# An attention and feed-forward kernel: the first w3 tile in two halves, and two w3 tiles multiplied with each quarter of wo

## The reference

```
def reference(q, k, v, centroids, moe_x..., moe2_x...):      # q, k, v: (2, 8, 768, 64)
    q_assign = argmax(norm(q) @ norm(centroids).T)           # 16 clusters per head
    k_assign = argmax(norm(k) @ norm(centroids).T)
    scores = where(q_assign == k_assign, q @ k.T / 8, -1e9)
    x = softmax(scores) @ v                                  # -> (1536, 512)
    h = ((x @ w1) * (x @ w2)) @ w3                           # w1, w2: (512, 1024), w3: (1024, 1024)
    x = h @ w_out                                            # w_out: (1024, 512), "wo" in the kernel
    h = x @ w_in                                             # (512, 2048)
    return (max(h, 0) + alpha * min(h, 0)) @ w_out2          # (1536, 512)
```

## Time and profile before

| | us |
|---|---|
| median of 3 runs | 747.94 (747.90 to 747.99) |
| the profiled execution, whole | 747.64 |
| its span, first to last instruction | 745.8 |
| PE busy in the span | 739.0 (99%) |
| DVE, ACT, POOL busy | 411.8, 311.6, 179.5 |

### The profile page before, as it was taken

How to read it: one execution, slowest core, us unless ns; L and a number is a source line. 1 busy time by engine, 2 the same in 40 slices (tenths; PEclk the granted TensorE clock), 3 DMA queues, 4 the chain that set the end, 5 groups by cost and what they waited for, 6 DMA issues and landing times.

```text
span 745.8 us, 10690 instructions
## 1 busy us (share of the span) xinstructions
PE 739.0 (99%) x3792; PEld 641.6 (86%) x3792; DVE 411.8 (55%) x632; ACT 311.6 (42%) x623; POOL 179.5 (24%) x211
## 2 busy tenths in 40 slices
PE   8999999999999999999999999999999999999998
PEld 6888999999999998888888888888888888888886
DVE  4435999999999984721311432575434333343432
ACT  5235988988988884311211422432012111121111
POOL 2141566866865893500000000000000000000000
PEclk9999999999999999999999999999999999999999
DMA  9636366566566233300000022140001000010001
GB/s 293 195 94 144 78 152 155 124 146 154 127 146 153 65 84 92 98 29 1 1 0 1 20 93 85 57 130 11 1 0 57 1 0 1 1 56 1 1 0 57
DMA packets 65371, 54.17 MB, mean 73 GB/s; under 512 B 32032, under 2 KB 54576, under 8 KB 65328
## 3 DMA queue, kind: packets, MB, share of 16 engines
q1 hardware_dynamic: 65328, 53.59, 27.9%
HBM read 31.50 MB, written 3.19 MB: 47 GB/s over the span
## 4 chain that ended last, share of the span: by engine, by line
PE 97%; DVE 1%; DMA 1%; ACT 1%; issue 0%; SPq 0%; DVEq 0%; ACTq 0%
PE slot L625 63%; PE acc L625 24%; PE slot L689 9%; PE acc L638 1%; PE slot L737 1%; DMA early<-in_moe_w_out 1%; DVE xl L1163 0%; DVE xl L1145 0%; ACT xh L938 0%; ACT xh L945 0%; DVE abx L1283 0%; DVE ab L1279 0%; ACT abx L1055 0%; ACT asb L1041 0%; ACT ost L1108 0%
## 5 line engine op out<-in xcount | busy, mean ns | idle before, releaser
L625 PE MATMUL slot<-xh,w 128*128 128x512 f32 x768 | 248.0, 389 | 0.0
L625 PEld LDWEIGHTS slot<-xh,w 128*128 128x128 f32 x768 | 144.1, 188 | 29.8
L625 PE MATMUL slot<-xl,w 128*128 128x512 f32 x384 | 149.4, 389 | 0.0
L1101 ACT CAST gh<-gf 128x512 fp32r<-128x512 f32 x48 | 29.9, 623 | 203.2 <-PE acc L625 186.0
L1206 DVE TENSOR_TENSOR pl<-slot,ph 128x384 fp32r<-128x384 f32 x192 | 97.6, 549 | 8.5 <-ACT ph L973 8.2
L1200 DVE TENSOR_REDUCE nm<-slot 128x1 f32<-128x768 f32 x96 | 91.4, 952 | 15.4 <-PE slot L625 13.8
L973 ACT CAST ph<-slot 128x384 fp32r<-128x384 f32 x192 | 83.5, 489 | 34.3 <-PE slot L689 33.8
L965 ACT ACTIVATE pf<-slot,nm 128x768 f32<-128x768 f32 x96 | 88.4, 921 | 4.6 <-DVE nm L1200 4.5
L625 PEld LDWEIGHTS slot<-xl,w 128*128 128x128 f32 x384 | 72.1, 188 | 15.0
L625 PE MATMUL slot<-k,q 80*128 80x384 f32 (+1 forms) x384 | 82.9, 337 | 0.0
L1329 DVE TENSOR_TENSOR gl<-gf,gh 128x512 fp32r<-128x512 f32 x48 | 33.2, 692 | 89.9 <-ACT gh L1101 89.9
(11 more groups left out here) (121 smaller groups left out, 1012.0 us busy)
## 6 DMA issues: line engine op xcount, KB each, us to landing
stage<-in_moe_w SPq DMA_DIRECT2D x16, 256.0 KB, 3.5
stage<-in_moe_w_in SPq DMA_DIRECT2D x16, 256.0 KB, 2.7
stage<-in_moe_w_out SPq DMA_DIRECT2D x16, 256.0 KB, 3.0
stage<-in_moe_w SPq DMA_DIRECT2D x6, 512.0 KB, 4.2
qk<-in_q SPq DMA_DIRECT2D x16, 192.0 KB, 3.9
qk<-in_k SPq DMA_DIRECT2D x16, 192.0 KB, 3.9
vn<-in_v SPq DMA_DIRECT2D x16, 192.0 KB, 3.8
q<-k SPq DMA_DIRECT2D x16, 192.0 KB, 3.8
```

What stands on the lines that cost most here:

```text
L625: return nc.tensor.matmul(o, a, b, start=start, stop=stop)
L1101: copy(gh[j % 2][:, :], gf[j % 2][:, :]).then_inc(gh_done, 1)
```

## The change

SP loads the first 512 columns of w3 tile 0 first of all, then the centroids, wo quarter 0, the other 512 columns, w3 tile 1, wo quarters 1 to 3, alpha, and the rest as before. PE turns tile 0 in two halves (`turn_first`), ACT and DVE split each half by itself (`first_hi_part`, `first_lo_part`), and ACT rounds wo quarter 0 in two instructions (`wo_first_hi`) with a semaphore of its own on the first. PE multiplies tile 0 with quarter 0, turns the second half and tile 1, and then multiplies tiles 0 and 1 with each quarter in turn. The transposes of the centroids and alpha move in front of the last quarter, and the scaling of the centroids on ACT behind the first rounding work. POOL clears `cwin` before it makes `ident`. There are 6 + 5 spins in place of 8 + 6.

```diff
--- before.py
+++ after.py
@@ -207,6 +207,8 @@
         low_in, join_in = ([sem(f"{name}{e}") for e in range(2)] for name in ("low_in", "join_in"))
         setup_pool, setup_act = sem("setup_pool"), sem("setup_act")
         cen_turned, table_done = sem("cen_turned"), sem("table_done")
+        ld_first, first_turned, first_hi, first_lo = (sem(name) for name in ("ld_first", "first_turned", "first_hi", "first_lo"))
+        wo_first = sem("wo_first")
         piece_hi, piece_lo = sem("piece_hi"), sem("piece_lo")
         front_hi, front_lo = sem("front_hi"), sem("front_lo")
         w3_turned, w3_hi, w3_lo = sem("w3_turned"), sem("w3_hi"), sem("w3_lo")
@@ -239,7 +241,7 @@
         NWO = NF // 2
         READY_W12, READY_W34 = NWO - W12_EARLY, NWO - W12_EARLY + NF
         W3_STAGED = 3
-        IDENT, ZEROS, OPERANDS = 2, 3, 5
+        ZEROS, IDENT, OPERANDS = 1, 3, 5
 
         def staged(e, piece):
 
@@ -381,13 +383,14 @@
                 if c % T6 == 4 and (not last or c // T6 + 2 < HB):
                     next_v(it, c // T6 + 2)
 
+            sp.dma_start(stage[0][:, 0:512], w3d[0][:, 0:512]).then_inc(ld_first, 16)
             sp.dma_start(cn[:, :], cen.rearrange("h c d -> (h c) d")).then_inc(ld_cen, 16)
-            load_w3(0, 0)
             load_wo(0)
-            sp.dma_start(al16, alpha.rearrange("(j p) -> j p", p=P)).then_inc(ld_al, 16)
+            sp.dma_start(stage[0][:, 512:1024], w3d[0][:, 512:1024]).then_inc(ld_stage[0], 16)
+            load_w3(1, 1)
             for i in range(1, NWO):
                 load_wo(i)
-            load_w3(1, 1)
+            sp.dma_start(al16, alpha.rearrange("(j p) -> j p", p=P)).then_inc(ld_al, 16)
             for f in (2, 3):
                 sp.dma_start(early[NWO + f - 2][:, :], w3d[f]).then_inc(ld_early[NWO + f - 2], 16)
             load_qk(0, 0)
@@ -453,10 +456,10 @@
                 ins.then_inc(setup_pool, 1)
                 pool.wait_ge(setup_pool, count[0])
 
+            ordered(nc.gpsimd.memset(cwin[0][:, :].bitcast(F32), 0.0))
             ordered(nc.gpsimd.memset(ident[:, :], 0.0))
             ordered(nc.gpsimd.affine_select(out=ident[:, :], in_=ident[:, :], compare_op=ALU.not_equal, fill=1.0,
                                             base=0, pattern=[[-1, P]], channel_multiplier=1))
-            ordered(nc.gpsimd.memset(cwin[0][:, :].bitcast(F32), 0.0))
             ordered(nc.gpsimd.memset(scl[:, :], 1.0))
             ordered(nc.gpsimd.memset(scl[0:D, :], SCALE))
             ordered(nc.gpsimd.memset(zero[:, :], 0.0))
@@ -747,19 +750,24 @@
                 if g == NF - 1:
                     last.then_inc(wc_full, 1)
 
-            def product_first():
-
-                o = slot[0][:, 0, :]
-                pe.wait_ge(piece_hi, 1)
-                pe.wait_ge(w3_hi, 1)
-                for g in range(2):
-                    mm(o, w3h[:, 0, g, :], woh[:, g, :], g == 0, False)
-                pe.wait_ge(piece_lo, 1)
-                for g in range(2):
-                    mm(o, w3h[:, 0, g, :], wol[:, g, :], False, False)
-                pe.wait_ge(w3_lo, 1)
-                for g in range(2):
-                    mm(o, w3l[:, 0, g, :], woh[:, g, :], False, False)
+            def turn_first(g0, ready, turned_to):
+
+                pe.wait_ge(ready, 16)
+                for g in range(g0, g0 + 4):
+                    last = nc.tensor.transpose(slot[1][:, g // 4, (g % 4) * P:(g % 4 + 1) * P],
+                                               stage[0][:, g * P:(g + 1) * P], ident[:, :])
+                last.then_inc(turned_to, 1)
+
+            def first_high(g):
+                mm(slot[0][:, 0, :], w3h[:, 0, g, :], woh[:, g, :], g == 0, False)
+
+            def first_low(g):
+                mm(slot[0][:, 0, :], w3l[:, 0, g, :], woh[:, g, :], False, False)
+
+            def first_cross(g):
+                last = mm(slot[0][:, 0, :], w3h[:, 0, g, :], wol[:, g, :], False, g == NF - 1)
+                if g == NF - 1:
+                    last.then_inc(wc_full, 1)
 
             def product_tile(f, parity):
                 pe.wait_ge(w3_lo, f + 1)
@@ -772,28 +780,45 @@
                     mm(slot[2][:, 1, 0:HS], cwin[0][:, 0:P], cwin[0][:, 0:HS], True, True)
 
             pe.wait_ge(setup_pool, ZEROS)
-            spin(8)
-            turn_w3(0, 0)
-            pe.wait_ge(setup_act, 1)
-            nc.tensor.transpose(acc[0:D, 0, 0:P], cn[:, :], ident[:, :])
-            pe.wait_ge(ld_al, 16)
-            nc.tensor.transpose(acc[:, 1, 0:NJ], al16, ident[0:NJ, 0:NJ]).then_inc(cen_turned, 1)
             spin(6)
-            product_first()
-            pe.wait_ge(piece_lo, 2)
-            product_wc(0, (2, 3))
-            pe.wait_ge(piece_lo, 3)
-            product_wc(0, (4, 5))
+            pe.wait_ge(setup_pool, IDENT)
+            turn_first(0, ld_first, first_turned)
+            spin(5)
+            pe.wait_ge(first_hi, 1)
+            pe.wait_ge(wo_first, 1)
+            first_high(0)
+            pe.wait_ge(piece_hi, 1)
+            first_high(1)
+            pe.wait_ge(first_lo, 1)
+            for g in range(2):
+                first_low(g)
+            turn_first(4, ld_stage[0], w3_turned)
+            pe.wait_ge(piece_lo, 1)
+            for g in range(2):
+                first_cross(g)
             turn_w3(1, 1)
-            pe.wait_ge(piece_lo, NWO)
-            product_wc(0, (6, 7))
-            turn_w3(2, 0)
             pe.wait_ge(w3_lo, 2)
-            product_wc(1, range(NF // 2))
+            product_wc(1, (0, 1))
+            for i in range(1, NWO):
+                if i == NWO - 1:
+                    pe.wait_ge(setup_act, 1)
+                    nc.tensor.transpose(acc[0:D, 0, 0:P], cn[:, :], ident[:, :])
+                    pe.wait_ge(ld_al, 16)
+                    nc.tensor.transpose(acc[:, 1, 0:NJ], al16, ident[0:NJ, 0:NJ]).then_inc(cen_turned, 1)
+                pe.wait_ge(piece_hi, i + 1)
+                for g in (2 * i, 2 * i + 1):
+                    first_high(g)
+                for g in (2 * i, 2 * i + 1):
+                    first_low(g)
+                pe.wait_ge(piece_lo, i + 1)
+                for g in (2 * i, 2 * i + 1):
+                    first_cross(g)
+                if i == NWO - 1:
+                    turn_w3(2, 0)
+                product_wc(1, (2 * i, 2 * i + 1))
             pe.wait_ge(table_done, 2)
             for half in range(2):
                 turned(0, 0, half, True)
-            product_wc(1, range(NF // 2, NF))
             for f in range(2, NF - 2):
                 turn_w3(f + 1, (f + 1) % 2)
                 for half in range(2):
@@ -929,9 +954,22 @@
             nc.scalar.activation(xf[0][:, 0, 0:D], cn[:, :], ACT.Square, accum_out=cs[:, 0:1]).then_inc(act_step, 1)
             act.wait_ge(dve_step, 1)
             nc.scalar.activation(cs[:, 2:3], cs[:, 1:2], ACT.Sqrt).then_inc(act_step, 1)
-            act.wait_ge(dve_step, CEN_DVE)
-            nc.scalar.mul(cn[:, :], cn[:, :], cs[:, 3:4]).then_inc(setup_act, 1)
-
+
+            def centroids_scaled():
+
+                act.wait_ge(dve_step, CEN_DVE)
+                nc.scalar.mul(cn[:, :], cn[:, :], cs[:, 3:4]).then_inc(setup_act, 1)
+
+            def first_hi_part(a, source, rounded):
+
+                act.wait_ge(source, 1)
+                copy(w3h[:, 0, 4 * a:4 * a + 4, :], slot[1][:, a, :].rearrange("p (g f) -> p g f", g=4)
+                     ).then_inc(rounded, 1)
+
+            def wo_first_hi():
+                act.wait_ge(ld_early[0], 16)
+                copy(woh[:, 0, :], early[0][:, 0:DM]).then_inc(wo_first, 1)
+                copy(woh[:, 1, :], early[0][:, DM:2 * DM]).then_inc(piece_hi, 1)
 
             def wo_hi(i):
                 act.wait_ge(ld_early[i], 16)
@@ -994,13 +1032,15 @@
                 if there(c):
                     probabilities(it, c)
 
+            first_hi_part(0, first_turned, first_hi)
+            wo_first_hi()
+            centroids_scaled()
+            first_hi_part(1, w3_turned, w3_hi)
+            w3_hi_part(1, 1)
+            wo_hi(1)
             act.wait_ge(setup_pool, OPERANDS)
-            wo_hi(0)
-            w3_hi_part(0, 0)
-            wo_hi(1)
             wo_hi(2)
             wo_hi(3)
-            w3_hi_part(1, 1)
             w3_hi_part(2, 0)
             wc_copy(0, 0)
             for half in range(2):
@@ -1158,6 +1198,12 @@
                     tt_(ctab[rows, :, col + NCL:col + 2 * NCL], turned_c, f32(ctab[rows, :, col:col + NCL]), ALU.subtract
                         ).then_inc(table_done, 1)
 
+            def first_lo_part(a, rounded, split):
+
+                dve.wait_ge(rounded, 1)
+                tt_(w3l[:, 0, 4 * a:4 * a + 4, :], slot[1][:, a, :].rearrange("p (g f) -> p g f", g=4),
+                    f32(w3h[:, 0, 4 * a:4 * a + 4, :]), ALU.subtract).then_inc(split, 1)
+
             def w3_lo_part(f, parity):
                 dve.wait_ge(w3_hi, f + 1)
```

(9 more changed lines are left out.)

## The result

| | before | after |
|---|---|---|
| median of 8 runs, us | 747.91 | 751.68 |
| lowest to highest | 747.35 to 748.06 | 749.23 to 754.08 |
| span of the profiled execution | 745.8 | 750.1 |
| start of product tile 2 (the yardstick) | 25.11 | 29.09 |

The change makes the kernel 0.5% slower: ratio 1.0053, 95% interval 1.0042 to 1.0064. The forecast was 748.3 us and no measurable change; the time lies above the top of its range, 750.9. Two things stand out before any row is read. The runs of after are 4.9 us apart, those of before 0.7. And nearly the whole loss of the profiled execution is there when product tile 2 starts: 3.98 us of 4.3. (The last 0.3 us lie behind it; I found no wait that holds them.)

A forecast was written before the change was run, and what follows sets the result against it. PE was taken as the bound, busy 739.0 of 745.8 us. S 12.1 + 12.9 + 0.45 gave the yardstick 25.45 against 25.11, so 747.94 + 0.35 = 748.3 us; range 747.1 to 750.9.

The forecast's parts named there:

- Where the time would be decided: PE's first 25 us: whatever it wins or loses there is carried to the end one for one.
- The landings: DMA queue at the start: centroids at 3.3 us, first wo quarter 5.0, w3 tile 1 near 8.0.
- The chain to S: Opening work through ACT, DVE and PE: 8.8 us from the centroids' landing to tile 1's first matmul.
- S: Time of PE's first matmul on w3 tile 1: forecast 12.1 us, range 11.7 to 12.4.
- c: Time when the centroids' load lands: forecast 3.3 us, range 2.9 to 3.5.
- From S to the yardstick: PE from tile 1's first matmul to product tile 2: 12.9 us of work plus a 0.45 us wait.
- q/k wait: PE at the second head's q/k transposes, waiting for freed accumulator halves: 0.45 us, from nothing to 0.75.
- The clock at S: PE's matmuls after its 2.4 us idle gap, taken at full pace, 0.228 us each: no clock loss.
- rival 1: Clock falls or isn't up at PE's gap; half pace up to 5 us costs 2.5 us, 750.8; chance 0.19.
- The page's rule: As cited beside rival 1: TensorE's clock gate is throttled by default, and activity releases it; no size given.
- Rival 2: Tile 1 really comes forward, set by its landing alone: yardstick -0.8 us, measurable at -1.5 us (746.4); chance 0.08.
- Rival 3: Change does nothing for the end: centroids at 2.9, no q/k wait, -0.5 us, 747.4; 0.73 together with the forecast.

The follow-up runs named there:

- e2: Changed kernel plus 12 spins (matmuls on zeros) behind the turn of w3 tile 1, filling PE's idle time: 749.02 us, ratio 1.0020 to the kernel before.
- e10: e1 with head 0's q/k transposes moved before tile 1's last 6 matmuls and the centroids' transposes one quarter earlier: 748.93 us.
- e11: e1 run once more unchanged, for comparison with e10 on the same chip: 749.22 us.
- e1: Changed kernel with 7 spins for 5 behind the first half tile and 12 spins behind the turn of w3 tile 1: 749.23 us.
- e8: Kernel before, with PE made to wait for wo's last quarter ahead of its first product, so it idles: 750.94 us.
- e9: e8 with 14 more spins in front of the added wait, so PE is not idle: 749.47 us.
- e3: Changed kernel with 7 spins for 5 behind the first half tile, nothing added later: 750.36 us.
- e12: e7 with both halves of the first w3 tile loaded ahead of wo's first quarter: 750.86 us.
- e4: e1 with the centroids' load back in front of the first half tile: 748.88 us.
- e6: e5 with wo's second quarter loaded, split and multiplied ahead of tile 1, and 6 late spins for 12: 749.65 us.
- e7: Changed kernel with w3 tile 1 loaded and multiplied after wo's last quarter as before, and 7 early spins for 5: 747.61 us, ratio 0.9996 to the kernel before.
- e5: e2 with head 0's q/k transposes moved before tile 1's last 6 matmuls and the centroids' transposes one quarter earlier: 750.48 us.

## Why the prediction was wrong

- **Where the time would be decided**: right. The yardstick carries 3.98 of 4.3 us, and behind it the kernels run alike.
- **The landings**: the centroids came at 3.66 for 3.3, the first wo quarter at 6.34 for 5.0, w3 tile 1 at 8.5 for 8.0. The second estimate failed: it counted the bytes ahead. The quarter took 4.7 us from its issue in both kernels though 256 KB less lay ahead of it; those 256 KB now came right behind it, at 2.12. With the same queue it took 3.8 to 5.4 us in other executions, so one trace of before could not give this time to 1 us. Where it was early (e2, e10) the chain hung on the centroids as forecast.
- **The chain to S**: the steps were right. In e2, the execution with the clock up early and the quarter early, the chain goes through the centroids and ACT, and S = 12.42 is c + 8.8 with c = 3.6. With the quarter at 4.7 us S was 12.77 (e11) and 12.80 (e1); in after it was 13.83, since the first products, the transposes and the cross terms before it ran at half pace. The 2.4 us wait was forecast as 2.4: it is the length of tile 1's own split on ACT and DVE, and moves with S.
- **From S to the yardstick**: 12.9 + 0.45 was forecast; e2 took 13.80. The q/k wait, read from start to start, was 0.6 in place of 0.45. The other 0.3 us are spread over the changes between matmuls and transposes and the restart at S, which I had left at nothing; no run takes them apart. In sum the forecast's path without any clock was 0.8 us short at the yardstick (26.22 in e2 for 25.45), and e2 lies 1.3 us over the kernel before, not 0.35. That alone would have been inside the range.
- **The clock at S, which the sum put at nothing**: this is the step that failed. The forecast had PE idle for 2.4 us and let the matmuls behind it go at full pace, 0.228 us each. They went at 0.43 us each for 3.1 us, and the fall cost 1.5 us (after against e1; the medians of e8 and e9 give 1.5 as well). The late rise, which the sum also left out, cost another 1.0.
- **The choice between forecast and rival 1**: the rival named the place (the gap before S) and the sign (matmuls over 0.4 us apart after 12 us). I gave it 0.19 against 0.73 because the gaps of up to 0.4 us in the earlier trace rows had cost no clock. They could not tell: the new gap was six times as long, and no row of before held one like it. Its price of 2.5 us is what the two slow stretches cost together, but that is luck: it was worked out as one stretch of 5 us behind S, and what came was 1.5 us behind S and 1.0 before it.
- **The range**: its top was forecast base plus one price, 748.3 + 2.5. The price held; the base did not (749.0 to 749.2 with the gap filled), and the sum left the range by 0.8 us.
- **The page's rule**: the Trainium skill, "TensorE: Matmul & The Clock Gate", Part 1, has the array throttled by default and released by activity. The traces agree, in both directions: the grant went to 0.50 within the idle time of e8 and back to 1.00 after some 6 us of renewed work.
- Rival 2 (early work comes forward) needed S at 10.7; nothing came near it. Rival 3 was not seen either.

## What to carry to other kernels

Work brought ahead of its inputs turns into an idle stretch on the bound engine, and on PE such a stretch costs more than its length: 2.4 us of waiting were followed by 3.4 us at the lower clock, which cost another 1.5 us, and by a spread of 5 us from execution to execution. A wait of 1.6 us did the same once (e3). Where a reordering moves a wait to PE, look up what stands in the gap, and if nothing does, put matmuls on zeros there or leave the order as it was. A wide spread with an unchanged page is a sign to read the distance between matmuls and the granted clock in short windows.

## What the runs showed of the hardware that I had not expected

- The rise of the clock moves between executions of nearly the same start. With first spins at 1.2 us, PE reached full pace by about 5 us (e2, e3, e12), between 6 and 8 (e1, e4, e6, e7, e10, e11) or only near 10 and 11 (after, e5). The two late ones both have 5 spins behind the first transposes, but so have e2 and e6; whether the two further spins matter isn't settled by these runs.
- A DMA's time to landing varies as well: wo's first quarter, third in the queue and issued at 1.65, took 3.8 to 5.4 us (e2, e10: 3.8 and 3.9; after: 4.7; e5: 5.4), and placed one transfer later (e12) 6.2. Why is open: it was never loaded alone.
- Waits and falls, as the traces have them: 0.8 and 1.0 us in e7 and no fall; 1.6 us in e3, 2.4 us in after and e3, 2.9 us in e8 and 3.2 us in e12, each with a fall. With the same program the fall can stay away: one of eight executions of after, three of seven of e3 and one of five of e12 have a mean grant of 1.000.
- The grant can fall while PE is still idle, or after it is back. In e8 it fell near 10.2 (PE back at 11.17), in after near 13.5 (13.83), in e12 near 7.9 (9.14), but in e3 near 8.2 with PE back at 7.56. It stayed at 0.50 for 3.4 us in after and both times in e3, 6.8 us in e8 and 10.2 us in e12. No run here shows what sets that length.
